# Attention fused with two mixture-of-experts layers: full rows for the last key tile, the row maxima turned by a matrix product, and work of the expert stage moved into attention

## What is computed

```python
# attention, per batch and head; S = 576, D = 64
scores = q @ k.T / sqrt(D) + minimum(-(cum[:, None] - cum[None, :]), 0)   # cum = cumsum(maximum(s, 0))
scores = where(causal, -1e9, scores)
attn   = exp(scores - max(scores)); attn = attn / (sum(attn) + 1e-9)
x      = attn @ v                          # laid out as 1152 x 512
# layer 1: logits = x @ w_gate + log1p(exp(x @ w_noise)) * noise; the best two experts, softmax of the two
# layer 2: P = exp(x @ w_gate2 - max), 8 rounds of row and column balancing
# an expert in either layer: y = relu(x @ w1[e]) @ w2[e], added with its token weight
```

## Time and profile before

| what | value |
|---|---|
| runs | 1268.42, 1271.45, 1346.13 us |
| median | 1271.45 us |
| profiled execution, its own time | 1267.45 us |
| its span, first to last instruction | 1265.7 us |
| granted TensorE clock, mean | 0.98 of full speed |
| busy share of PE / weight loads / DVE / ACT / POOL | 96% / 86% / 39% / 29% / 12% |

### The profile page before, as it was taken

The page is one execution under the profiler, slowest core; times in us unless marked ns, Lnnn a source line. Parts: engine busy times, 40 slices in busy tenths (PEclk is TensorE's granted clock), DMA queues, the critical chain, the costliest instruction groups (busy, mean ns, idle before and its releaser), DMA issues.

```text
span 1265.7 us, 17437 instructions
## 1 busy us (share of the span) xinstructions
PE 1220.8 (96%) x6613; PEld 1082.7 (86%) x6613; DVE 491.4 (39%) x1089; ACT 361.0 (29%) x680; POOL 150.1 (12%) x220
## 2 busy tenths in 40 slices
PE   8999479999999889999999999999999999999998
PEld 5888368888888778999999999999999999999997
DVE  5553765555554551443133233233224224224311
ACT  4555324444444331122122122122113113112110
POOL 7664221000011450000000000000000000000000
PEclk9999679999999979999999999999999999999999
DMA  6672314444555532011011012002101101100000
GB/s 154 161 180 89 143 50 173 170 172 177 179 179 180 165 109 100 1 67 67 1 67 66 0 33 99 0 0 81 51 0 66 66 0 66 66 0 0 25 25 25
DMA packets 23829, 102.97 MB, mean 81 GB/s; under 512 B 4464, under 2 KB 9072, under 8 KB 19824
## 3 DMA queue, kind: packets, MB, share of 16 engines
q1 hardware_dynamic: 17360, 85.97, 20.5%
q0 software_dynamic: 3360, 11.01, 3.0%
q10 hardware_dynamic: 3072, 5.51, 1.3%
HBM read 87.75 MB, written 10.30 MB: 77 GB/s over the span
## 4 chain that ended last, share of the span: by engine, by line
PE 93%; DVE 3%; DMA 2%; ACT 1%; issue 1%; POOL 1%; SPq 0%; POOLq 0%; DVEq 0%
PE bank L701 14%; PE bank L700 14%; PE bank L699 14%; PE bank L681 13%; PE bank L683 13%; PE bank L682 13%; PE bank L616 4%; PE bank L569 1%; PE bank L600 1%; PE bank L601 1%; PE bank L622 1%; PE bank L733 1%; DMA x_sb<-x_dram,gather_at 1%; PE bank L581 1%; PE bank L645 0%
## 5 line engine op out<-in xcount | busy, mean ns | idle before, releaser
L681 PE MATMUL bank<-xTh,w1h 128*128 128x384 f32 (+1 forms) x1024 | 343.3, 335 | 3.0 <-DVE xTl L1091 1.6
L682 PE MATMUL bank<-xTl,w1h 128*128 128x384 f32 (+1 forms) x1024 | 340.8, 333 | 0.0
L683 PE MATMUL bank<-xTh,w1l 128*128 128x384 f32 (+1 forms) x1024 | 340.7, 333 | 0.0
L909 ACT ACTIVATE hh<-bank 128x384 fp32r<-128x384 f32 (+1 forms) x256 | 123.1, 481 | 654.7 <-PE bank L683 654.7
L701 PE MATMUL bank<-w2h,hl 128*128 128x512 f32 (+1 forms) x768 | 302.3, 394 | 0.0
L700 PE MATMUL bank<-w2l,hh 128*128 128x512 f32 (+1 forms) x768 | 300.6, 391 | 0.0
L699 PE MATMUL bank<-w2h,hh 128*128 128x512 f32 (+1 forms) x768 | 300.0, 391 | 0.0
L1111 DVE SCALAR_TENSOR_TENSOR hl<-bank,hh 128x384 fp32r<-128x384 f32 (+1 forms) x256 | 139.4, 544 | 367.2 <-ACT hh L909 367.1
L681 PEld LDWEIGHTS bank<-xTh,w1h 128*128 128x128 f32 x1024 | 193.9, 189 | 5.5 <-issue 2.1
L682 PEld LDWEIGHTS bank<-xTl,w1h 128*128 128x128 f32 x1024 | 194.1, 190 | 1.2
L683 PEld LDWEIGHTS bank<-xTh,w1l 128*128 128x128 f32 x1024 | 193.8, 189 | 0.0
(11 more groups left out here) (168 smaller groups left out, 685.0 us busy)
## 6 DMA issues: line engine op xcount, KB each, us to landing
raw<-in_w SPq DMA_DIRECT2D x15, 2048.0 KB, 8.1
raw<-in_w1b SPq DMA_DIRECT2D x8, 2048.0 KB, 7.6
raw<-in_w2b SPq DMA_DIRECT2D x8, 2048.0 KB, 7.7
k_raw<-in_kT SPq DMA_DIRECT2D x16, 288.0 KB, 5.3
y_dram<-x_sb ACTq DMA_DIRECT2D x16, 256.0 KB, 4.1
q_raw<-in_qT SPq DMA_DIRECT2D x8, 288.0 KB, 6.3
q_two<-w2l SPq DMA_DIRECT2D x8, 288.0 KB, 3.1
x_dram<-x_sb SPq DMA_DIRECT2D x1, 2304.0 KB, 7.8
```

What stands on the lines that cost most here:

```text
L681: pe.matmul(dst, w1h[:, c, fs], xTh[:, c, ts], start=(c == 0), stop=False)
L682: pe.matmul(dst, w1h[:, c, fs], xTl[:, c, ts], start=False, stop=False)
L683: mm = pe.matmul(dst, w1l[:, c, fs], xTh[:, c, ts], start=False, stop=(c == DC - 1))
L909: act.activation(hh[:, f, 0:n_cols], bank[:, f % UP_BANKS, 0:n_cols], ACT.Relu).then_inc(st.hh_ready, 1)
```

## The change

Part by part:

1. **Last key tile.** The unused 64 rows of `probT` and `v_sb` for the last key tile are set to zero once, on DVE, and all products of `mix` read 128 rows. DVE counts `pad_ready`; PE waits for `pad_ready` 3 ahead of its warm-ups.
2. **Maxima.** `aug` gets a fourth column (zeros) and becomes fp32r; `turn_max` is a matmul with `ident_r`, an fp32r copy of the identity that DVE makes and that is the third count of `pad_ready`. q_top and k_top have 68 rows.
3. **POOL's order.** In each step the mask comes ahead of the low part, and `LOW_AHEAD` is 13.
4. **w1l.** Eight halves (128x512) on POOL, one after each mask of steps 71 to 78. For this `k_top` gets a space of its own.
5. **Gates.** The six operations stand in DVE's queue after step 60.
6. **Four token tiles** are transposed after the mixes of steps 76 to 79; step 76 waits for `head_done` 15 first. DVE takes the low parts of tiles 0 to 2 ahead of the last `finish`.
7. **raw2** now shares space with attention's buffers and is loaded behind the store of x; xTh and xTl lie beyond attention's space.

```diff
@@ SBUF
-        AUG = HD + 3
+        AUG = HD + 4
-        k_top = [w1l_flat[0:AUG, i * N:(i + 1) * N] for i in range(HEADS_RING)]
+        k_top_all = sb("k_top", [AUG, HEADS_RING, N], F32R, where=attn)
+        k_top = [k_top_all[:, i, :] for i in range(HEADS_RING)]
...
-        K_HIGH_AHEAD, Q_HIGH_AHEAD, LOW_AHEAD = 18, 17, 14
+        K_HIGH_AHEAD, Q_HIGH_AHEAD, LOW_AHEAD = 18, 17, 13
+        W1_LOW_AT, EARLY_AT, GATES_AT = 71, 76, 60
+        EARLY = ST
@@ SP
-            sp.dma_start(raw2[:], w2[0]).then_inc(SP_.raw2_loaded, 16)
-
             sp.wait_ge(head_done, G)
             sp.dma_start(noise_sb[:], noise).then_inc(noise_loaded, 16)
 
             sp.dma_start(x_dram.rearrange("(t p) d -> p t d", p=P), x_sb[:]).then_inc(x_stored, 16)
+            sp.dma_start(raw2[:], w2[0]).then_inc(SP_.raw2_loaded, 16)
@@ POOL
-            pool.memset(aug[:], 1.0).then_inc(aug_ready, 1)
+            pool.memset(aug[:, :, :, 0:3].bitcast(F32), 1.0).then_inc(aug_ready, 1)
+            pool.memset(aug[:, :, :, 3:4].bitcast(F32), 0.0).then_inc(aug_ready, 1)
...
+            def low_w1(c, half):
+                cols = slice(half * F // 2, (half + 1) * F // 2)
+                pool.wait_ge(SP_.w1h_ready, c + 1)
+                part = pool.tensor_tensor(w1l[:, c, cols], raw1[:, c, cols], w1h[:, c, cols].bitcast(F32), ALU.subtract)
+                if half:
+                    part.then_inc(SP_.w1_ready, 1)
+
             for k in range(-LOW_AHEAD, ALL):
+                if k >= 0:
+                    cut(k)
                 h, c = low_at(k)
                 if h is not None:
                     low_part(h, c, k)
-                if k >= 0:
-                    cut(k)
+                if k >= W1_LOW_AT and k - W1_LOW_AT < 2 * DC:
+                    low_w1((k - W1_LOW_AT) // 2, (k - W1_LOW_AT) % 2)
...
-            pool.wait_ge(scores_ready, ALL)
-            for c in range(DC):
-                pool.wait_ge(SP_.w1h_ready, c + 1)
-                if c:
-                    pool.wait_ge(SP_.w1_ready, c)
-                pool.tensor_tensor(w1l[:, c, :], raw1[:, c, :], w1h[:, c, :].bitcast(F32), ALU.subtract).then_inc(SP_.w1_ready, 1)
@@ PE
-                    mm = pe.transpose(bank[0:3, MAX_AT, at:at + rows], aug[0:rows, n % MAX_RING, t, :], ident[0:rows, 0:rows])
+                    mm = pe.matmul(bank[0:4, MAX_AT, at:at + rows], aug[0:rows, n % MAX_RING, t, :], ident_r[0:rows, 0:rows],
+                                   start=True, stop=True)
...
                 for j in range(t + 1):
-                    wide = rows_in(j)
                     at = PROB_AT[j] + (t - j) * P
                     mm = pe.matmul(bank[rows, OUT_AT + n % 2, t * (HD + 1):(t + 1) * (HD + 1)],
-                                   probT[0:wide, n % UNIT_RING, at:at + nrow],
-                                   v_sb[0:wide, w, j, (HD + 1) * b:(HD + 1) * (b + 1)], start=(j == 0), stop=(j == t))
+                                   probT[:, n % UNIT_RING, at:at + nrow],
+                                   v_sb[:, w, j, (HD + 1) * b:(HD + 1) * (b + 1)], start=(j == 0), stop=(j == t))
...
             pe.wait_ge(const_ready, 6)
+            pe.wait_ge(pad_ready, 3)
             for _ in range(WARM_UPS):
                 keep_warm(BANK)
             for k in range(-ROUGH_AHEAD, ALL):
...
                 if k >= 0:
                     mix(k)
+                if k >= EARLY_AT:
+                    if k == EARLY_AT:
+                        pe.wait_ge(head_done, G - 1)
+                    turn_token(SP_, k - EARLY_AT, x_sb)
...
-            for t in range(2 * BLK_T):
+            for t in range(EARLY, 2 * BLK_T):
                 turn_token(SP_, t, x_sb)
@@ DVE
             link(v.memset(zeros_g[0:G, :], 0.0))
+            v.memset(probT[HALF:P, :, PROB_AT[ST]:PROBS], 0.0).then_inc(pad_ready, 1)
+            v.memset(v_sb[HALF:P, :, ST, 1:1 + P], 0.0).then_inc(pad_ready, 1)
             v.wait_ge(s_loaded, 16)
...
             v.tensor_copy(k_top[0][0:HD, :], k_raw[0:HD, 0, :]).then_inc(k_first, 1)
             v.wait_ge(const_ready, 6)
-            v.wait_ge(aug_ready, 1)
+            v.tensor_copy(ident_r[:], ident[:]).then_inc(pad_ready, 1)
+            v.wait_ge(aug_ready, 2)
...
                 if k >= STEPS and k % STEPS == 0:
                     finish(unit_of(k) - 1)
+                if k == GATES_AT:
+                    split_gates()
+            for t in range(BLK_T):
+                token_low(SP_, t)
             finish(G - 1)
```

More of the change, by code:

```diff
@@ L622, in keep_warm @@
                 pe.matmul(bank[:, BANKS - 1, 0:cols], ones[:], causal[:, 0:cols], start=True, stop=True)
-            pe.wait_ge(const_ready, 6)
-            for _ in range(WARM_UPS):
-                keep_warm(BANK)
-            for k in range(-ROUGH_AHEAD, ALL):
-                if k + ROUGH_AHEAD < ALL:
-                    rough(k + ROUGH_AHEAD)
-                if k < -SCORES_AHEAD:
-                    keep_warm(BANK // 2)
-                for n, part in turns_at(k):
-                    turn_max(n, part)
-                if 0 <= k + SCORES_AHEAD < ALL:
-                    scores(k + SCORES_AHEAD)
-                if k >= 0:
-                    mix(k)
             def turn_token(st, t, src):
@@ L1066, in finish @@
                                 ALU.mult).then_inc(head_done, 1)
-            for k in range(-ROUGH_AHEAD, ALL):
-                if k + ROUGH_AHEAD < ALL:
-                    row_max(k + ROUGH_AHEAD)
-                if k >= STEPS and k % STEPS == 0:
-                    finish(unit_of(k) - 1)
-            finish(G - 1)
-            v.wait_ge(head_done, G)
             def split_w1(st, n):
@@ L1085, in token_low, with split_gates @@
                                 xTh[:, :, ts].bitcast(F32), ALU.subtract).then_inc(st.xTl_ready, 1)
+            def split_gates():
+                v.wait_ge(gates_loaded, 48)
+                for which, (cn, c0, g0) in enumerate(((2 * E, 0, 0), (E, 2 * E, 4 * E))):
+                    high, low = gate_w[:, :, g0:g0 + cn], gate_w[:, :, g0 + cn:g0 + 2 * cn]
+                    link(v.tensor_copy(high, gates[:, :, c0:c0 + cn]))
+                    link(v.tensor_tensor(low, gates[:, :, c0:c0 + cn], high.bitcast(F32), ALU.subtract))
+                    link(v.tensor_tensor(fold[which][:], ident[0:2 * cn, 0:cn], ident[0:2 * cn, cn:2 * cn], ALU.add))
+                assert count[0] == GATES_SPLIT, count[0]
+            for k in range(-ROUGH_AHEAD, ALL):
+                if k + ROUGH_AHEAD < ALL:
+                    row_max(k + ROUGH_AHEAD)
+                if k >= STEPS and k % STEPS == 0:
+                    finish(unit_of(k) - 1)
+                if k == GATES_AT:
+                    split_gates()
+            for t in range(BLK_T):
+                token_low(SP_, t)
+            finish(G - 1)
+            v.wait_ge(head_done, G)
             def gathered_low(n):
@@ L1144, in dense @@
                 dense_expert(st, m, acc_tiles, E - 1, follows)
-            v.wait_ge(gates_loaded, 48)
-            for which, (cn, c0, g0) in enumerate(((2 * E, 0, 0), (E, 2 * E, 4 * E))):
-                high, low = gate_w[:, :, g0:g0 + cn], gate_w[:, :, g0 + cn:g0 + 2 * cn]
-                link(v.tensor_copy(high, gates[:, :, c0:c0 + cn]))
-                link(v.tensor_tensor(low, gates[:, :, c0:c0 + cn], high.bitcast(F32), ALU.subtract))
-                link(v.tensor_tensor(fold[which][:], ident[0:2 * cn, 0:cn], ident[0:2 * cn, cn:2 * cn], ALU.add))
-            assert count[0] == GATES_SPLIT, count[0]
-            for t in range(NT):
+            for t in range(BLK_T, NT):
                 token_low(SP_, t)
```

52 lines of the change are left out of this document (34 added, 18 removed).

## The result

The changed kernel takes 1341.24 us (median of 1340.14, 1341.0, 1341.47, 1341.7), the kernel before beside it 1268.42, 1271.45, 1272.07 and 1346.13. The ratio is 1.0554, 95% interval 1.0533 to 1.0576: slower by 70 us, where 1268 was forecast. In some runs TensorE's clock falls early in attention and stays low there, so ratios compare only runs within 1.5% of the fastest of the same kernel; where the clock always fell these are all runs, and in g3, g5 and h2 some of them lost it for a part.

The account below looks back on a forecast made before the run. The prediction took PE to bound attention and the experts, with slack only at the start and in the routing behind attention. Terms +6.7 - 3.3 + 0 - 1.4 + 2.0 - 5.0 = -1.0 gave 1266.5, with 1.5 for the median 1268; range 1259 to 1278.

Parts of the forecast that it names:

- Whole-percent changes have no source in these sums: Whole kernel: 2% (25 us) would need a stage outside attention to change or a disturbed median; within 2%: chance 0.96.
- C: Maxima in attention by an fp32r product instead of transposes: 0, bounds -2.9 to +2.1.
- A: Start: warm-ups wait for ident_r, so rough(0) comes 7.7 late, 1.0 given back: +6.7, bounds +5.5 to +8.3.
- B: Full 128 rows in the mix's last two passes of each unit, 0.20 saved in each: -3.3, bounds -2.2 to -3.7.
- D: POOL's mask ahead of the low part, so PE's mix waits less at heads' first units: -1.4, bounds 0 and -2.4.
- E: Gates at step 60: operations held up beside POOL delay a maximum PE needs: +2.0, bounds 0 to +3.4.
- F: Behind attention: shorter chain from last mix to gate rows' turn, less attention's longer end: -5.0, ends -7.6 and -1.0.
- G: Loads of raw2 and raw1 behind x: 0, a delay up to 2 us being in the range.
- 1, the late start hidden: Start: loads and high parts bound it, so the late start costs near 1; time 1262, chance 0.15.
- 2, POOL as the bound at attention's end: Steps 72 to 79: masks behind halves of w1l come 3 to 4 us later, all on PE; time 1274, chance 0.2.
- 3, full clock behind attention and gates unheld: Behind attention the clock stays full (-7.3) and gates cost 0; time 1263.7, chance 0.2.
- slower: Whole kernel slower by over 2%: chance 0.03.

Follow-up runs that it names:

- g3: Changed kernel with pad_ready's wait behind the warm-ups, filling products at steps -3 and 4, and one more fp32 product per unit: 1264.95 us, ratio 0.9987.
- g5: Changed kernel with pad_ready's wait behind the warm-ups, filling products at steps -3 and 4, and POOL's old order: 1279.11 us, ratio 1.0036.
- h2: Kernel before with its maxima turned by the fp32r product, every product made twice: 1273.52 us, ratio 1.0047.
- e3: Changed kernel, late start kept, with the maxima turned by fp32 transposes again: 1271.66 us, ratio 1.0019.
- f1: Kernel before with only the fp32r product for its maxima, the identity's wait behind the warm-ups: 1342.44 us, ratio 1.056.
- e2: Kernel before with only the late start added (ident_r made, PE waits for it ahead of its warm-ups): 1277.82 us, ratio 1.007.
- e1: Changed kernel with the wait for pad_ready moved behind the nine warm-up products: 1336.31 us, ratio 1.0543.
- g4: Changed kernel with transposes, pad_ready's wait behind the warm-ups, filling products at steps -3 and 4, and gates at step 67: 1262.48 us, ratio 0.9951.
- f3: Changed kernel, product kept, with pad_ready's wait behind the warm-ups and one filling product of 512 columns at step 4: median 1286.74 us.
- h1: Kernel before with its maxima turned by a plain fp32 product in place of a transpose: 1279.81 us, ratio 1.0082.
- g2: Changed kernel with transposes, pad_ready's wait behind the warm-ups, and filling products of 512 columns at steps -3 and 4: 1263.25 us, ratio 0.9954.
- i1: g4 with 64 unused bytes ahead of the turned tokens (xTh, xTl): 1259.48 us, ratio 0.9923.
- e4: Changed kernel, late start and product kept, with the mix reading 64 rows of the last key tile again: 1346.01 us.
- f4: Kernel before with one more warm-up product of 512 columns at step 4, ahead of the scores: 1273.85 us, ratio 1.0021.
- f2: Changed kernel with transposes for the maxima and the wait for pad_ready behind the warm-ups: 1263.77 us, ratio 0.9947.
- i2: Kernel before with 64 unused bytes ahead of xTh and 64 behind xTl: ratio 1.0084, 1278.9 to 1280.1 us where the clock held.

## Why the prediction was wrong

The step that failed was "Whole-percent changes have no source in these sums". They had one: the granted clock in attention, which I took from the earlier trace rows as given (1.00 from 30 to 122 us), though one of the three runs, 1346.13, stood 75 us above the others. I called that a disturbed median. In the other 36 slow runs of the kernel before (1339 to 1350) the mean granted clock was 0.91 to 0.92 against 0.98, so it was in all likelihood this very effect, and its price, read straight from the list of runs, was the one to use: 71 us by the traces (the last mix at 202.83 against 134.68 in e3, which lacks the product's gain of 2.7). In the terms of the sum the step is C, the product of the maxima: it stood at 0 with bounds from -2.9 to +2.1, and alone it cost 5.6% in f1, 71 us. The prediction named the clock only behind attention and in the experts.

The terms, with full clock, were within their bounds for the most part:

- **A, forecast +6.7 (5.5 to 8.3): 7.9 in e2, 6.9 in the changed kernel** (first mix at 30.43 against e1's 23.56). `ident_r` ended at 10.14 (10.1 forecast), rough(0) came at 19.81 (19.9). "I give 1.0 back" was a little too much: 0.6 came back in e2. The wait of 0.95 for the doubled k is gone there, but one of 0.55 stands in its place. The two figures differ mostly by the warm-ups, 10.34 us in e2 and 9.52 in the changed kernel.
- **B, -3.3 (-2.2 to -3.7): -2.1.** A unit takes 6.53 (g4) where two took 13.55, that is 6.78; by pairs of units 0.49 went, of which 0.23 is D's. The remaining 0.13 a unit is just the part inside the step, as in the lower bound; "the next product's late start" stayed. B and D weren't measured apart.
- **C, 0 (-2.9 to +2.1): -2.7 at full clock**, 6.53 to 6.36 a unit (f3). What failed is the duration: I read "an fp32r product of the same 128 columns" as 0.11 from a product behind others, but three turned in a row take 0.18, 0.06 each. The reading of the 64 rows was right: two turns should take 0.09 by that and take 0.18, so the switch costs 0.09 with the product too. The Trainium skill (TensorEngine Tiling (Array Packing), Key Properties) says that a change of tiling mode drains TensorE; these runs agree in that the loss stays with the product, 0.09 us. And the 2.7 us that the edit saves are PE work whose loss, by h1 and h2, is at least a part of what cost 70.
- **D, -1.4: about -1.5.** The 0.23 at a head's first unit is gone: the full units behind the first take 6.53 to 6.57 in g4, but for one of 6.75.
- **E, +2.0 (0 to 3.4): +0.8 to +1.0.** The unit from step 60 took 7.30 in g2 and 7.55 in e3, with one wait of PE for `aug` (0.6 in g2). That DVE's queue would make PE wait for a maximum was right, the size wasn't: of the six operations one was held up, not three (the longest took 0.87 us in e3 and 0.66 in g2, the others 0.15 to 0.27), so the six took 2.0 and 1.8 us, not 3.7. At step 67 the wait is gone.
- **F, -5.0 (-7.6 to -1.0): -6.7.** From the start of the last mix's last pass to the gate rows' turn it is 10.0 us in e3, g4 and the changed kernel, 18.7 before; attention's last unit is 2.07 longer (5.14 in e3 against 3.07, forecast 2.0). I forecast 7.3 for full clock and took a middle; the clock held there in all of them (it is 1.00 from 201.16 to 214.8 in the changed kernel). The low parts of tokens beside POOL's halves took 0.69 us as elsewhere, so these weren't held. Chain after, against the earlier trace rows:

```profile
204.91 1.09 PE bank L637 x8
...
212.81 2.23 PE bank L661 x18
```

- **G, 0: loads cost nothing**, but the same part of the change (space for buffers) costs +4.0 in the second expert layer by the tokens' place (i1), a term the sum lacked.

Summed, 7.9 - 2.1 - 2.7 - 1.5 + 1.0 - 6.7 + 4.0 = -0.1: at full clock the change would have been no change. That this is near the forecast's -1.0 is luck: C, D, E and F came out 5.5 us better than forecast, A, B and the tokens' place 6.4 worse. Without C the sum is +2.6; e3, which has all but C, measured +2.4 by its ratio (0.5 to 4.3).

The rivals: 1, the late start hidden, fell by e2. 2, POOL as the bound at attention's end, came close. From step 72 on POOL has no idle time in e3 and g4, and the chain of waits of e3 runs through it:

```profile
131.08 1.24 POOL w1l L492
132.33 0.26 POOL probT L486
...
132.63 1.10 PE bank L622 x8
```

But PE waited only once, 0.2 us, for a mask (its weight loads three times, 0.9 us together), and not the 3 to 4 us of the rival, so it fell. 3, full clock behind attention and gates unheld, was right on F and nearly on the gates, though E wasn't 0. The case that happened, with its sign, wasn't among them; "slower" had 0.03.

What is shown and what isn't: shown is that the product alone takes the clock (f1), that transposes give it back (e3), that filling the wait at head 2's load ends the falls of the kernel before (0 of 12, against 8 of 17 beside it; with both waits filled, 0 of 18 in g2, g4 and i1), and that doing the product twice holds the clock in seven of 13 runs. Not settled is the rest: h2's six losses of 13 against 5 of 19 for the kernel before, which may be chance, and that three of them were partial, of which the kernel before had none in 90. There the kind of work may count beside its amount. Nor do the traces give a rule by which a profile that loses the clock could be told from one that holds it: e3 and e4 look alike ahead of it, and i1 held it with a unit drawn out from 6.5 to 7.3 us.

## What to carry to other kernels

Before changing PE's stream in a stretch that just holds full clock, look at the list of runs: a run far above the others with the same work can be the price tag for losing the clock, and its mean granted clock tells (0.91 against 0.98 here); if so, the stretch is near the edge. There, an edit that saves PE work can cost more than it saves; count what is taken out around the longest waits, and put a product that nobody reads into the wait (f4's last mix came 0.5 us later for it and the whole kernel took 2.7 more by its ratio, and four of ten runs were spared 75). And when buffers move, compare the mean duration of the long loops before and after: a shift of one buffer by 64 bytes was worth 4 us here.

## What the runs showed of the hardware

- The clock of attention has two courses, which in most runs separate early. At 2.4 GHz a unit takes 6.4 to 7.5 us, at 1.2 GHz 11.6 to 12.2. In the eight profiles in which it fell, it came back only at attention's end (at the earliest 9.6 us ahead of the last pass, in f2; at 201.16 in the changed kernel), though PE was busy 160.00 of 160.00 us. In f3, whose loss was smaller, it fell later, at 95.97, and was back at 143.75; the other runs with a partial loss (g5, h2, e4) have no profile.
- The Trainium skill (TensorE: Matmul & The Clock Gate, Part 4: PE-mode transpose) says, of bf16 transposes in one kernel, that the fast clock doesn't engage for them. By that, products in their place would have made the clock safer; here it was the reverse, e3 with transposes 1271.66, the changed kernel with products 1341.24. The measurement decides: the transposes of these tiles, among the other products of attention, served the clock better than the single fp32r product; against the fp32 product of h1 (fell in 0 of 5, the kernel before in 5 of 19) no difference is shown.
- A turn of 128 columns takes 0.11 us as an fp32 transpose, 0.06 as an fp32r product; going to 64 rows costs 0.09 in either.
- Up products of 384 columns took 338 ns in g4 and 335 in i1, with the tokens moved by 64 bytes, no wait and nothing else changed. In the older layout (i2) the opposite move left them at 334 and drew out the down products of `hh` from 388 to 394 ns.
